# Attention scores on two row tiles of the TensorE array: q without zero rows, the two heads' products next to each other

## The chip, the cores and the metric

One Trainium2 chip; the kernel runs on 1 of its cores as one launch. The metric is the device time of that launch in microseconds (us). Engines by their names in the profile: PE is TensorE (matrix products), PEld its weight loads, DVE is VectorE, ACT is ScalarE, POOL is GpSimd, and SP is the engine that issues nearly all DMAs here.

## The reference

Three stages follow each other. The change touches the first.

```python
# q, k, v: batch 4, 8 heads, 768 rows, head size 64, f32; n_sink 4, window 128
scores = scale * np.matmul(q, k.transpose(0, 1, 3, 2))
keep = is_sink | in_window             # the first 4 keys, and the last 128
scores = np.where(keep, scores, -1e9)
a = np.exp(scores - max);  a = a / (sum + 1e-9)
x = a @ v                              # -> 3072 tokens x 512
# dense layer: h = x @ w_in; y = (h * cos(h)) @ w_out      (512 -> 2048 -> 512)
# routing to one of 8 experts, then relu(y @ w1[e]) @ w2[e], times its gate
```

## The kernel before

The 32 heads are worked in 16 pairs. Both heads of a pair lie on top of each other: the 128 partitions of `k_sb` hold k transposed of head 0 in partitions 0 to 63 and of head 1 in 64 to 127. `qz` holds q transposed twice as wide, `[128, 2, 768]`: in the part for head 0 the partitions 64 to 127 are zero, in that for head 1 the partitions 0 to 63. So each head's scores are a product over all 128 partitions, half of whose terms are zero. The zeros are written once by two DVE memsets (L793), and the loads (L395) put the values beside them, one DMA for each head.

A pair has six steps, i = 0 to 5, one for each block of 128 query rows. A step computes scores against the block's own keys and the block before (128 columns for i = 0, 256 else), and for i from 2 on against 32 sink columns too ("wide" steps, 288 columns). The order on PE is written out by hand in `attention` (L1247): the scores of step n (L1185, sinks L1187), then, where there are sinks to add, the turn of the packed sink probabilities of step n-3 (L1205), the turn of the probabilities of step n-2 (L1197), the product with v of step n-3 (L1219), and the sink product (L1230). The last two sorts fall in steps i = 0 and i = 2. A matrix product in f32 shows as two MATMULs in the trace, each with a weight load of its own (192 score products of 128 or 256 columns, 384 MATMULs); a turn shows as one.

L1219 works on half of the array's columns: head 0 fills the 64 output partitions 0 to 63, head 1 those from 64 on (128*64 in the trace). All other products of this stage use the whole array (128*128).

DVE in step n: the denominators and reciprocals of step n-1 (L861, L863) as soon as ACT's two exponentials of that step are done, scaling of its first head (L865), masking with row maximum of step n (L839, one for each head), in steps i = 0 and 2 the copy of the turned sinks (L854), the copy of the turned probabilities of step n-2 (L847), and in steps i = 2 and 5 half of a weight split for the next stage (L872). ACT in step n: scaling of the second head of step n-1 (L623), two exponentials (L606), in i = 1 and 4 a weight split (L593), in odd steps the copy of a finished block (L618).

Scores go to three PSUM banks in turn, so the scores of head h of step n wait until the mask of three products earlier has read its bank (`masked_made`). SP loads a pair's k, q, v and four sink pieces of v (L391 to L403) once the sinks of that buffer's last pair are weighed (step i = 2 of the pair after it), and PE takes them up three steps later, at i = 0 (`qkv_loaded`).

Of the kernel before, what the change touches and what calls it, by code (L numbers as in the profile page):

```python
# [24 lines left out]
P = 128  # L25
# [6 lines left out]
def at_least(engine, semaphore, value):  # L32

    if isinstance(value, int) and value <= 0:
        return
    engine.wait_ge(semaphore, value)


def build_program(nc, qT, kT, v, config, w_dense, modality, w_gate, modality_bias, w_expert, out):
    PAIRS, _, S = qT.shape  # L40
    HD = 64
# [4 lines left out]
    SINK = 32  # L46
# [16 lines left out]
    STEPS = 2 * QB  # L63
# [9 lines left out]
    with ctx:  # L73
        def sb(name, shape, dt=F32, where=ctx):
            return where.enter_context(nc.sbuf_tensor(name, shape, dt))

        def sem(name):
            return ctx.enter_context(nc.semaphore(name))
# [21 lines left out]


        with ExitStack() as a:
            qz = [sb(f"qz{i}", [P, 2, S], where=a) for i in range(2)]
            k_sb = [sb(f"k_sb{i}", [P, S], where=a) for i in range(2)]
            v_sb = [sb(f"v_sb{i}", [P, QB, P], where=a) for i in range(2)]
            v_sink = [sb(f"v_sink{i}", [P, 2 * P], where=a) for i in range(2)]
            x_stage = [sb(f"x_stage{i}", [P, S], where=a) for i in range(2)]
            masked = [sb(f"masked{i}", [P, 2, WIDE], where=a) for i in range(2)]
            probs = [sb(f"probs{i}", [P, 2, WIDE], where=a) for i in range(4)]
            probsT = [sb(f"probsT{i}", [P, 2, 2 * P], where=a) for i in range(2)]  # L110
            sink_probs = [sb(f"sink_probs{i}", [P, 4, SINK], where=a) for i in range(2)]
            sink_probsT = sb("sink_probsT", [P, P], where=a)
            neg_max = sb("neg_max", [P, 2 * STEPS], where=a)
            sums = sb("sums", [P, 2 * STEPS], where=a)
            den = sb("den", [P, 2 * STEPS], where=a)
            rden = sb("rden", [P, 2 * STEPS], where=a)

            rel, below, keep = (x_stage[0][:, 2 * P * i:2 * P * (i + 1)] for i in range(3))
            col, is_sink = (x_stage[1][:, P * i:P * (i + 1)] for i in range(2))
            mask0 = sb("mask0", [P, P], where=a)  # L120
            mask1 = sb("mask1", [P, 2 * P], where=a)
            mask2 = sb("mask2", [P, 2 * P + SINK], where=a)
# [100 lines left out]
        ident_cleared = sem("ident_cleared")  # L223
        consts_made = sem("consts_made")
        mask_step = sem("mask_step")
        q_zeros_made = sem("q_zeros_made")
        sink_zeros_made = sem("sink_zeros_made")
        qkv_loaded = [sem(f"qkv_loaded{i}") for i in range(2)]
        raw_loaded = [sem(f"raw_loaded{i}") for i in range(2)]
# [2 lines left out]
        scores_done = sem("scores_done")  # L232
        masked_made = sem("masked_made")
# [115 lines left out]
        def columns_of(i):  # L349

            return (P, 2 * P) if i == 0 else (0, 2 * P if i == 1 else WIDE)
# [6 lines left out]
        S_BANK, T_BANK, O_BANK, X_BANK = bank[0:3], bank[3:5], bank[5:7], bank[7]  # L358
# [13 lines left out]
        def _(sp):  # L372
# [14 lines left out]
            def load_pair(it, i):  # L387

                at_least(sp, sinks_weighed, 2 * SG * (it - 1) + SG * (i + 1))
                pair = 2 * it + i  # L390
                sp.dma_start(k_sb[i][:, :], kT[bass.ds(pair, 1), :, :].rearrange("o p s -> (o p) s")).then_inc(qkv_loaded[i], 16)  # L391
                if isinstance(it, int) and it == 0:
                    sp.wait_ge(q_zeros_made, i + 1)
                for h in range(2):
                    sp.dma_start(qz[i][HD * h:HD * (h + 1), h, :],  # L395
                                 qT[bass.ds(pair, 1), HD * h:HD * (h + 1), :].rearrange("o p s -> (o p) s"),
                                 ).then_inc(qkv_loaded[i], 16)
                sp.dma_start(v_sb[i][:, :, :].rearrange("p n d -> p (n d)"),
                             v[bass.ds(pair, 1), :, :].rearrange("o p s -> (o p) s")).then_inc(qkv_loaded[i], 16)
                if isinstance(it, int) and it == 0:  # L400
                    sp.wait_ge(sink_zeros_made, i + 1)
                for u in range(4):
                    sp.dma_start(v_sink[i][SINK * u:SINK * (u + 1), HD * u:HD * (u + 1)],  # L403
                                 v[bass.ds(pair, 1), 0:SINK, HD * (u % 2):HD * (u % 2 + 1)].rearrange("o p s -> (o p) s"),
                                 ).then_inc(qkv_loaded[i], 16)
                load_piece(it, i)
# [73 lines left out]
        def _(pool):  # L480
# [34 lines left out]
                    pack_all(it)  # L515
            with pool.Else():
                for i in range(2):
                    pool.wait_ge(qkv_loaded[i], 128)
                pool.memset(any_q[:, :, :], 0.0).then_inc(any_zeros, 1)
                pool.iota(any_rel[:, :], pattern=[[-1, S]], base=0, channel_multiplier=1,  # L520
                          allow_small_or_imprecise_dtypes=True).then_inc(any_zeros, 1)
                pool.iota(any_sink[:, :], pattern=[[1, S]], base=0, channel_multiplier=0,
                          allow_small_or_imprecise_dtypes=True).then_inc(any_zeros, 1)
# [259 lines left out]
        def _(dve):  # L783
# [5 lines left out]
                ins.then_inc(mask_step, 1)  # L789
                dve.wait_ge(mask_step, done[0])  # L790

            for i in range(2):
                dve.memset(qz[i][:, :, :], 0.0).then_inc(q_zeros_made, 1)  # L793
            dve.wait_ge(config_loaded, 16)
            halves = cfg_lo[:, :].rearrange("p (a b) -> p a b", b=2)
            dve.tensor_copy(halves[:, :, 0:1], cfg_i[:, :].bitcast(U32).rearrange("p (a b) -> p a b", b=2)[:, :, 0:1]).then_inc(mask_step, 1)
# [218 lines left out]
            n = link(dve.tensor_scalar(chain2[:, :], chain2[:, :], 1.0, None, ALU.min))  # L1015
            after(n)
            for m, x in enumerate((bsel, bpart)):
                n = link(dve.tensor_tensor(x, bias_sb[:, m:m + 1, :].broadcast_to(full), wide(is_mod[:, m, :], full), ALU.mult))
# [25 lines left out]
            n = link(dve.tensor_tensor(weighed[:, :, :], logits[:, :, :], wide(top[:, :], full), ALU.is_equal))  # L1044
# [9 lines left out]
            def by_tile(x):  # L1054
# [14 lines left out]
            n = link(dve.tensor_reduce(in_use[:, 0::2, :].rearrange("p a e -> p e a"),  # L1069
                                       over[:, :, :].rearrange("p e (i a) -> p e a i", a=2), AX.X, ALU.add))  # L1070
# [102 lines left out]
        def _(pe):  # L1173

            def scores(it, n):
                par, i = n // QB, n % QB
                if i == 0:
                    pe.wait_ge(qkv_loaded[par], 128 * it + 128)
                for h in range(2):

                    at_least(pe, masked_made, 2 * STEPS * it + 2 * n + h - 2)
                    to = S_BANK[(2 * n + h) % 3]
                    q = qz[par][:, h, i * P:(i + 1) * P]
                    lo, hi = columns_of(i)
                    last = pe.matmul(to[:, lo:2 * P], q, k_sb[par][:, (i - 1) * P + lo:(i + 1) * P], start=True, stop=True)  # L1185
                    if hi > 2 * P:
                        last = pe.matmul(to[:, 2 * P:hi], q, k_sb[par][:, 0:SINK], start=True, stop=True)  # L1187
                    last.then_inc(scores_done, 1)

            def turn_probs(it, m):  # L1190
                pe.wait_ge(scaled_first, STEPS * it + m + 1)
# [324 lines left out]
```

## Time and profile before

| | |
|---|---|
| median of 3 runs | 1204.07 us (1203.34 to 1204.21) |
| profiled execution, span | 1203.8 us |
| attention | 8.85 us (first scores) to about 256 us |
| dense layer | from 260.2 us |
| PE busy over the span | 1145.4 us (95%) |
| granted TensorE clock, mean | 0.978 |

The span, from the first to the last instruction, is all that the profile has of its execution's time; the median of the timed runs stands 0.3 us above it. All times in the rows below are microseconds from the start of the span. "Idle before <-releaser" is how long the engine had nothing to do before such an instruction, and what ended that.

### The profile page before, as it was taken

What the parts mean: (1) busy time and instruction counts of PE and PEld (TensorE: products, weight loads), DVE (VectorE), ACT (ScalarE), POOL (GpSimd) and SP (SyncE); (2) the same over time, 40 slices, a digit from 0 to 9 for tenths busy, and PEclk for the clock granted to TensorE, in tenths of its full rate; (3) what the DMA queues carried; (4) which work ended last, traced back from release to release, by engine and by line L of the source; (5) the groups of instructions that cost most, each with busy time, mean ns of one, the idle gap of its engine ahead of it and who ended that gap; (6) DMA issues with size and microseconds to landing.
All of it is one profiled execution on the core that took longest, in us unless ns stands there. A gap on an engine that the chain in (4) does not pass through costs nothing.

```text
span 1203.8 us, 20823 instructions
## 1 busy us (share of the span) xinstructions
PE 1145.4 (95%) x6588; PEld 961.5 (80%) x6589; DVE 618.9 (51%) x1522; ACT 493.6 (41%) x1099; POOL 86.7 (7%) x174
## 2 busy tenths in 40 slices
PE   6999999989999999999999999997599999999996
PEld 5777777768888888888888888886589999899895
DVE  7888888854454444444345445445773222252221
ACT  5777777753333333333334334332352221241221
POOL 0000000000000000000000000000111121221121
PEclk9999999989999999999999999998599999999998
DMA  5444444510001002002002000000573111121110
GB/s 118 143 142 142 142 142 142 173 67 1 1 9 63 1 0 70 0 0 70 0 0 70 0 0 36 1 1 35 193 257 111 35 52 36 36 105 52 35 50 18
DMA packets 33993, 76.61 MB, mean 64 GB/s; under 512 B 10398, under 2 KB 10398, under 8 KB 33952
## 3 DMA queue, kind: packets, MB, share of 16 engines
q1 hardware_dynamic: 29312, 63.50, 17.1%
q0 software_dynamic: 4640, 12.59, 3.1%
q8 instruction: 22, 0.36, 0.1%
q14 instruction: 19, 0.16, 0.0%
HBM read 58.77 MB, written 19.92 MB: 65 GB/s over the span
## 4 chain that ended last, share of the span: by engine, by line
PE 86%; DVE 4%; issue 3%; DMA 3%; SPq 2%; ACT 1%; POOL 0%; DVEq 0%; POOLq 0%; ACTq 0%
PE bank L1310 23%; PE bank L1324 22%; PE bank L1450 14%; PE bank L1438 12%; PE bank L1185 4%; DMA v_sink<-v_n 3%; PE bank L1219 2%; PE bank L1230 2%; PE bank L1197 2%; PE bank L1342 1%; PE bank L1420 1%; SPq L403 1%; PE bank L1411 1%; SPq L395 1%; PE bank L1187 1%
## 5 line engine op out<-in xcount | busy, mean ns | idle before, releaser
L1310 PE MATMUL bank<-x_hi,w_hi 128*128 128x512 f32 x384 | 156.1, 406 | 4.7 <-issue 4.2
L1310 PE MATMUL bank<-x_lo,w_hi 128*128 128x512 f32 x384 | 153.0, 399 | 0.0
L1310 PE MATMUL bank<-x_hi,w_lo 128*128 128x512 f32 x384 | 152.7, 398 | 0.0
L1324 PE MATMUL bank<-w_hi,g_hi 128*128 128x512 f32 x384 | 152.3, 397 | 0.4 <-DVE g_lo L986 0.4
L1324 PE MATMUL bank<-w_hi,g_lo 128*128 128x512 f32 x384 | 152.1, 396 | 0.0
L1324 PE MATMUL bank<-w_lo,g_hi 128*128 128x512 f32 x384 | 151.8, 395 | 0.0
L1145 DVE SCALAR_TENSOR_TENSOR h_lo<-bank,h_hi 128x256 fp32r<-128x256 f32 x112 | 47.6, 425 | 173.4 <-ACT h_hi L756 172.2
L1450 PE MATMUL bank<-xg_hi,w_hi 128*128 128x256 f32 x448 | 127.7, 285 | 4.3 <-DVE xg_lo L1139 2.8
L974 DVE TENSOR_SCALAR whole<-turns 128x512 f32<-128x512 f32 x96 | 41.0, 427 | 175.4 <-ACT turns L707 175.4
L1185 PE MATMUL bank<-k_sb,qz 128*128 128x256 f32 (+1 forms) x384 | 114.7, 400 | 16.8 <-DMA v_sink<-v_n 16.8
L707 ACT ACTIVATE turns<-bank 128x512 f32<-128x512 f32 x96 | 57.5, 599 | 177.7 <-PE bank L1310 177.7
L1450 PE MATMUL bank<-xg_hi,w_lo 128*128 128x256 f32 x448 | 128.1, 286 | 0.0
L1450 PE MATMUL bank<-xg_lo,w_hi 128*128 128x256 f32 x448 | 127.6, 285 | 0.0
L756 ACT ACTIVATE h_hi<-bank 128x256 fp32r<-128x256 f32 x112 | 43.2, 386 | 187.1 <-PE bank L1450 182.0
L606 ACT ACTIVATE probs<-masked,neg_max 128x288 f32<-128x288 f32 (+1 forms) x192 | 96.5, 503 | 35.1 <-DVE neg_max L839 25.3
L712 ACT ACTIVATE cosine<-frac 128x512 f32<-128x512 f32 x96 | 60.7, 632 | 114.2 <-DVE frac L977 114.2
L986 DVE TENSOR_TENSOR g_lo<-g_sb,g_hi 128x512 fp32r<-128x512 f32 x96 | 66.5, 693 | 65.0 <-ACT g_hi L717 64.5
L982 DVE TENSOR_TENSOR g_sb<-bank,cosine 128x512 f32<-128x512 f32 x96 | 66.4, 692 | 64.0 <-ACT cosine L712 63.5
L1450 PEld LDWEIGHTS bank<-xg_hi,w_hi 128*128 128x128 f32 x448 | 85.7, 191 | 9.4 <-issue 5.6
L1310 PEld LDWEIGHTS bank<-x_hi,w_hi 128*128 128x128 f32 x384 | 72.9, 190 | 21.3 <-issue 4.4
L717 ACT ACTIVATE g_hi<-g_sb 128x512 fp32r<-128x512 f32 x96 | 60.7, 632 | 71.1 <-DVE g_sb L982 71.1
L1450 PEld LDWEIGHTS bank<-xg_lo,w_hi 128*128 128x128 f32 x448 | 86.0, 192 | 3.5
(159 smaller groups left out, 2087.8 us busy)
## 6 DMA issues: line engine op xcount, KB each, us to landing
raw<-w_expert SPq DMA_DIRECT2D x32, 512.0 KB, 4.9
raw<-w_dense SPq DMA_DIRECT2D x16, 512.0 KB, 4.5
k_sb<-k_t SPq DMA_DIRECT2D x16, 384.0 KB, 3.3
qz<-q_t SPq DMA_DIRECT2D x32, 192.0 KB, 4.0
v_sb<-v_n SPq DMA_DIRECT2D x16, 384.0 KB, 4.4
xT_scratch<-x_stage SPq DMA_DIRECT2D x16, 384.0 KB, 4.6
x_raw<-xT_scratch SPq DMA_DIRECT2D x6, 1024.0 KB, 5.1
y_scratch<-y_sb SPq DMA_DIRECT2D x6, 1024.0 KB, 4.3
```

The source lines that it names most:

```text
L606: act.activation(probs[n % 4][:, h, lo:hi], masked[n % 2][:, h, lo:hi], ACT.Exp, scale=-1.0, bias=neg_max[:, 2 * n + h:2 * n + h + 1], acc ...
L707: act.activation(turns[:, :], H_BANK[f % 2][:, :], ACT.Copy, scale=INV_2PI, bias=0.25).then_inc(turns_made, 1)
L712: act.activation(cosine[:, :], frac[:, :], ACT.Sin, scale=TWO_PI).then_inc(cos_made, 1)
L717: act.activation(g_hi[f % 4][:, :], g_sb[:, :], ACT.Copy).then_inc(g_hi_made, 1)
L982: dve.tensor_tensor(g_sb[:, :], H_BANK[f % 2][:, :], cosine[:, :], ALU.mult).then_inc(g_made, 1)
L986: dve.tensor_tensor(g_lo[f % 4][:, :], g_sb[:, :], g_hi[f % 4][:, :].bitcast(F32), ALU.subtract).then_inc(g_lo_made, 1)
L1145: dve.scalar_tensor_tensor(out=h_lo[f % 4][:, :], in0=EH_BANK[f % 2][:, 0:TT], scalar=0.0, in1=h_hi[f % 4][:, :].bitcast(F32), op0=ALU.max ...
L1185: last = pe.matmul(to[:, lo:2 * P], q, k_sb[par][:, (i - 1) * P + lo:(i + 1) * P], start=True, stop=True)
L1310: last = pe.matmul(H_BANK[f % 2][:, :], a[:, w], b[:, k, :], start=x == 0, stop=x == 3 * KD - 1)
L1324: last = pe.matmul(Y_BANK[t][:, :], a[f % 4][:, t * P:(t + 1) * P], b[:, w], start=f == 0 and x == 0, stop=f == FB1 - 1 and x == 2)
L1438: last = pe.matmul(EY_BANK[j][:, :], a[f % 4][:, j * P:(j + 1) * P], b[:, w], start=f == 0 and x == 0, stop=f == FB2 - 1 and x == 2)
L1450: last = pe.matmul(EH_BANK[f % 2][:, 0:TT], a[:, w], b[:, k, :], start=x == 0, stop=x == 3 * KD - 1)
```

## The change

`qz` becomes `q_sb`, `[128, 768]`: each head's q in its own 64 partitions, loaded by one DMA. The two memsets go, and with them the wait of SP for them. Each head's product now contracts over its own 64 partitions, the weights and the moving operand both taken from those: head 0 on rows 0 to 63 of the array, head 1 on rows 64 to 127. Both heads' window products are issued, then both heads' sink products. The wait for a free bank stands once, ahead of both heads: for the mask of head 0 of the step before.

```diff
-            qz = [sb(f"qz{i}", [P, 2, S], where=a) for i in range(2)]
+            q_sb = [sb(f"q_sb{i}", [P, S], where=a) for i in range(2)]
...
-                if isinstance(it, int) and it == 0:
-                    sp.wait_ge(q_zeros_made, i + 1)
-                for h in range(2):
-                    sp.dma_start(qz[i][HD * h:HD * (h + 1), h, :],
-                                 qT[bass.ds(pair, 1), HD * h:HD * (h + 1), :].rearrange("o p s -> (o p) s"),
-                                 ).then_inc(qkv_loaded[i], 16)
+                sp.dma_start(q_sb[i][:, :], qT[bass.ds(pair, 1), :, :].rearrange("o p s -> (o p) s")).then_inc(qkv_loaded[i], 16)
...
-            for i in range(2):
-                dve.memset(qz[i][:, :, :], 0.0).then_inc(q_zeros_made, 1)
...
-                    pe.wait_ge(qkv_loaded[par], 128 * it + 128)
+                    pe.wait_ge(qkv_loaded[par], 112 * it + 112)
+                at_least(pe, masked_made, 2 * STEPS * it + 2 * n - 1)
+                lo, hi = columns_of(i)
+                to = [S_BANK[(2 * n + h) % 3] for h in range(2)]
+                rows = [slice(HD * h, HD * (h + 1)) for h in range(2)]
+                last = [None, None]
                 for h in range(2):
-
-                    at_least(pe, masked_made, 2 * STEPS * it + 2 * n + h - 2)
-                    to = S_BANK[(2 * n + h) % 3]
-                    q = qz[par][:, h, i * P:(i + 1) * P]
-                    lo, hi = columns_of(i)
-                    last = pe.matmul(to[:, lo:2 * P], q, k_sb[par][:, (i - 1) * P + lo:(i + 1) * P], start=True, stop=True)
-                    if hi > 2 * P:
-                        last = pe.matmul(to[:, 2 * P:hi], q, k_sb[par][:, 0:SINK], start=True, stop=True)
-                    last.then_inc(scores_done, 1)
+                    last[h] = pe.matmul(to[h][:, lo:2 * P], q_sb[par][rows[h], i * P:(i + 1) * P],
+                                        k_sb[par][rows[h], (i - 1) * P + lo:(i + 1) * P], start=True, stop=True)
+                if hi > 2 * P:
+                    for h in range(2):
+                        last[h] = pe.matmul(to[h][:, 2 * P:hi], q_sb[par][rows[h], i * P:(i + 1) * P],
+                                            k_sb[par][rows[h], 0:SINK], start=True, stop=True)
+                for h in range(2):
+                    last[h].then_inc(scores_done, 1)
```

PE, a step i = 2 with its sinks, before: head 0 (window, sinks), then head 1, and behind them the rest of the step. The size is that of the output, partitions by columns; a row is one product.

```order
L1185 MATMUL bank<-k_sb,qz 128x256 [waits masked_made]
L1187 MATMUL bank<-k_sb,qz 128x32
L1185 MATMUL bank<-k_sb,qz 128x256 [waits masked_made]
L1187 MATMUL bank<-k_sb,qz 128x32
L1205 MATMUL bank<-ident,sink_probs 128x128 [waits sinksT_made,sinks_packed]
L1197 MATMUL bank<-ident,probs 128x128 [waits probsT_made,scaled_second,scaled_first]
L1197 MATMUL bank<-ident,probs 128x128
L1219 MATMUL bank<-probsT,v_sb 64x128 [waits probsT_made]
L1219 MATMUL bank<-probsT,v_sb 64x128 x3
L1230 MATMUL bank<-sink_probsT,v_sink 128x128 [waits sinksT_made]
```

The same step now (L1177 and L1181 are the scores; L1193, L1201, L1215, L1226 the rest):

```order
L1177 MATMUL bank<-k_sb,q_sb 128x256 [waits masked_made]
L1177 MATMUL bank<-k_sb,q_sb 128x256
L1181 MATMUL bank<-k_sb,q_sb 128x32 x2
L1201 MATMUL bank<-ident,sink_probs 128x128 [waits sinksT_made,sinks_packed]
L1193 MATMUL bank<-ident,probs 128x128 [waits probsT_made,scaled_second,scaled_first]
L1193 MATMUL bank<-ident,probs 128x128
L1215 MATMUL bank<-probsT,v_sb 64x128 [waits probsT_made]
L1215 MATMUL bank<-probsT,v_sb 64x128 x3
L1226 MATMUL bank<-sink_probsT,v_sink 128x128 [waits sinksT_made]
```

The second head's window product has moved ahead of the first head's sink product, one of the two waits is gone, and nothing behind the scores has moved.

SP, the load of a pair in the loop, before:

```order
L391 ISA [waits sinks_weighed]
L391 DMA k_sb<-k_t 128x768
L395 DMA qz<-q_t 64x768
L395 ISA
L395 DMA qz<-q_t 64x768
L398 DMA v_sb<-v_n 128x768
L403 DMA v_sink<-v_n 32x64
```

And now:

```order
L390 ISA [waits sinks_weighed]
L390 DMA k_sb<-k_t 128x768
L391 DMA q_sb<-q_t 128x768
L392 DMA v_sb<-v_n 128x768
L397 DMA v_sink<-v_n 32x64
```

One DMA with both heads stands in the place of two, and everything behind it is one issue earlier.

## Rows read from the trace of the kernel before

**Rows 1.** The page: busy time, and one line of the 40 slices.
```profile
PE 1145.4 (95%) x6588; PEld 961.5 (80%) x6589; DVE 618.9 (51%) x1522; ACT 493.6 (41%) x1099; POOL 86.7 (7%) x174
...
DVE  7888888854454444444345445445773222252221
```

**Rows 2.** Stretches: PE, PEld, DVE, ACT, POOL busy; clock; DMA share; GB/s.
```profile
40.00:240.00 200.00, 191.00 (x1520) 154.14 (x1519) 178.07 (x682) 147.95 (x458) 12.39 (x52) 1.00 0.48 143
258.00:268.00 10.00, 7.79 (x22) 6.18 (x23) 1.12 (x2) 2.21 (x3) 2.02 (x12) 0.66 0.38 122
```

**Rows 3.** Waits from 40 to 240 us, DVE: us in total, times, longest.
```profile
DVE masked L839 <- PE bank L1185: 4.9, 16, 0.5
DVE masked L839 <- PE bank L1187: 2.5, 13, 0.2
```

**Rows 4.** Waits from 40 to 240 us, PE.
```profile
PE bank L1185 <- DMA v_sink<-v_n: 7.5, 12, 1.3
PE bank L1230 <- DVE sink_probsT L854: 1.4, 4, 0.5
```

**Rows 5.** Chain, steps i = 1 and i = 2 on PE: start, us, what.
```profile
101.94 0.87 PE bank L1185 x4
102.81 0.44 PE bank L1197 x4
103.24 0.59 PE bank L1219 x8
103.83 0.63 PE bank L1185 x2
104.46 0.14 PE bank L1187 x2
104.60 0.51 PE bank L1185 x2
105.11 0.14 PE bank L1187 x2
105.25 0.14 PE bank L1205
...
106.20 0.72 PE bank L1230 x4
```

**Rows 6.** Timeline of PE: a product with v of two blocks only.
```profile
245.55 0.44 PE L1219 MATMUL bank<-probsT,v_sb 128*64 128x128 f32 x4
245.92 0.70 PE L1185 MATMUL bank<-k_sb,qz 128*128 128x256 f32 x2
```

**Rows 7.** Chain, from one wide step's denominators to the next's.
```profile
18.04 0.18 DVE den L861
...
19.22 1.16 ACT probs L606 x4
20.40 0.18 DVE den L861
```

**Rows 8.** Chain at the start of the kernel.
```profile
1.12 1.35 DVE qz L793
...
2.48 0.57 SPq L395
...
3.72 0.59 SPq L398
...
5.75 3.05 DMA v_sink<-v_n
```

**Rows 9.** Timeline of SP at the start: start, us, what.
```profile
1.18 0.42 SPq L391 DMA_DIRECT2D k_sb<-k_t  x1
```

**Rows 10.** Timeline of SP, a pair's load in the loop.
```profile
107.10 0.33 SPq L391 DMA_DIRECT2D k_sb<-k_t  x1
107.53 1.19 SPq L395 DMA_DIRECT2D qz<-q_t  x2
```

**Rows 11.** Chain, the end of that load.
```profile
110.98 3.54 DMA v_sink<-v_n
```

More of the change, by code:

```diff
@@ L225, in build_program @@
         mask_step = sem("mask_step")
-        q_zeros_made = sem("q_zeros_made")
         sink_zeros_made = sem("sink_zeros_made")
@@ L517, in _ @@
                 for i in range(2):
-                    pool.wait_ge(qkv_loaded[i], 128)
+                    pool.wait_ge(qkv_loaded[i], 112)
                 pool.memset(any_q[:, :, :], 0.0).then_inc(any_zeros, 1)
```

## The prediction, made before the changed kernel ran

> **What bounds the kernel now.** I read the busy line and the slices first [rows 1]: PE is busy 95% of the span, but in the first eight slices, the attention, DVE stands at 7 to 8 tenths and falls to 4 behind them. So a shorter PE there is not simply a shorter kernel. The stretch from 40 to 240 us says it in numbers [rows 2]: PE busy 191.0 of 200 us, DVE 178.1, ACT 148.0, at full granted clock. PE is the longest, DVE has 11% left.
>
> Next the waits. DVE waited for scores 4.9 us in 16 waits for L1185 and 2.5 us in 13 for L1187, together 7.4 us in 200 [rows 3]. That is what late scores cost DVE. PE itself waited 7.5 us for a pair's load and 1.4 us for DVE's copy of the sinks [rows 4]. Both engines wait for each other a little: the stage is balanced, not plainly PE-bound. The wide steps show the third bound, a loop through two engines: denominators of one step, reciprocal, scaling, mask, two exponentials (1.16 us), denominators of the next, from 18.04 to 20.40 = 2.36 us [rows 7], with PE nowhere in it. A pair of six steps takes about 15.2 us now ((256 - 8.85) / 16 less the last steps' tail); six such loops would be 14.2 us, and DVE's weight split and sink copies lengthen some of them. So even with PE for nothing a pair could lose 1 us at most, 16 us in all.
>
> **What the scores cost on PE, part by part.** In step i = 1 the four score MATMULs of 256 columns take 0.87 us, 0.217 each; the four turns of 128 columns 0.44, 0.11 each [rows 5]. In a wide step the first head takes 0.63 + 0.14, the second 0.51 + 0.14, together 1.42 us [rows 5]. Two MATMULs of 256 columns would be 0.43. The first head's 0.63 holds 0.20 more: it follows L1219, which uses half of the columns, and the array has to be empty before its division changes, with the weight load bare behind it. The second head's 0.51 holds 0.08: its weight load had only the 32-column product to hide under. A sink product's 0.14 is the bare load of its second weights.
>
> Do two tiles of the array work at the same time? The trace has them in columns. L1219 has 8 MATMULs of 128 columns, and takes 0.59 us, not 8 x 0.11 = 0.88 [rows 5]; with 4 it takes from 245.55 to 245.92, 0.37 [rows 6]. The difference is 0.22 for four more MATMULs, so two slots of 0.11: both heads run side by side, and what is left over, 0.59 - 0.43 = 0.37 - 0.22 = 0.15, is the change of division. If rows do as columns do, a wide step's scores take what one head takes: 0.63 + 0.14 = 0.77, and 0.65 us is saved; in i = 1 0.43, in i = 0 0.22 (by 128 columns). Per pair 4 x 0.65 + 0.43 + 0.22 = 3.25 us.
>
> The Trainium skill speaks to this in "TensorE: Matmul & The Clock Gate", "Part 3: Packing small matmuls": matmuls start and end in strict program order. By that rule head 1's first pass could only start with head 0's second, and two passes of two heads would take three slots, not two; L1219 with 4 MATMULs would then take 0.15 + 3 x 0.11 = 0.48. The trace has 0.37 [rows 6] and disagrees, for column tiles. I keep the rule as a rival for row tiles.
>
> **What is added on PE.** Before, scores and turns used the same division, and the turn's weights loaded under the scores. Now the array changes its division behind the scores in all six steps, and ahead of the scores also in the two steps that follow a sink product (i = 1 and 3); in the others L1219 stands ahead, whose change is paid already. No row shows a change from or to a division by rows. The nearest are 0.20 (columns to whole) and 0.15 (whole to columns) [rows 5]. Bounds: nothing, and twice 0.20. I take 0.20, less the 0.08 that the turn's load costs bare behind a sink product already: 4 x 0.12 + 2 x 0.20 behind, 2 x 0.20 ahead, 1.28 us per pair. PE's net: 3.25 - 1.28 = 1.97 us less per pair, some 13.2 of 15.2.
>
> In "TensorEngine Tiling (Array Packing)", "Key Properties", the Trainium skill states that changing the tiling mode drains the engine. The 0.20 behind L1219 agrees [rows 5]; a price for rows it does not give.
>
> **What of it reaches the end.** Only what DVE and ACT waited for. The 7.4 us of waits stand in 200 us, the attention has 242: 9.0 us. Those for L1187 (2.5) are the wide steps' second head, whose scores now come 0.65 us earlier: all of it goes. Those for L1185 (4.9) are steps i = 0 and 1, where head 0's scores are the late ones. Head 0 needs its own two passes as before, 0.43 us at i = 1, and now 0.20 more ahead of them. What helps there is only that PE comes to them earlier, from its slack. Both ends: none of it, all of it. I take a quarter, 1.2, since the entry stands against it and the load of the pair keeps PE late at i = 0. Then 3.7 us of 200, 4.5 us of 242. Ends for this term: 2.5 x 1.21 = 3.0 and 9.0.
>
> The bank wait. Head 0's scores now wait for the mask of head 0 of the step before, not for one mask earlier. That mask ends long before: behind it PE has turns, L1219 and mostly more, at least 1.03 us [rows 5]. Cost nothing; behind it would stand everything on PE. Had PE no such work, it would be 0.5 us a step.
>
> **The loads.** SP issues one q DMA for two. In the loop two take 1.19 us [rows 10], so about 0.6 us goes; k's, of 128 partitions, takes 0.33. The last sink piece lands 3.54 us after SP is done [rows 11], and the whole chain, 107.10 to 114.52, is 7.4 us against three steps i = 3 to 5. It becomes 6.8, while those three steps get shorter by some 0.3. PE waits for it now [rows 4], with DVE mostly at work meanwhile. Taken at nothing, 0 to 1.5 us gain. The bytes are the same.
>
> At the start it counts. k's issue ends at 1.60 [rows 9]; the first q issue waits for the memset until 2.48 [rows 8]. It can now start at 1.64, 0.84 earlier, and one issue of 0.57 + 0.04 is gone: 1.45 us. The rest of the chain, v, the sink pieces and 3.05 us of landing [rows 8], moves with it. Late next would be DVE's masks; they start earlier too, by up to the second memset, and had over 1 us to spare. From there the attention runs in its loop, so I count all of it: 1.45 us, at worst 0.8.
>
> **Sum.** 1203.8 (span) - 4.5 - 1.45 = 1197.85; the median of the timed runs stands 0.3 above the span: 1198.1 us. By the ends of the terms: 1203.8 - 3.0 - 0.8 + 0.3 = 1200.3, and 1203.8 - 9.0 - 1.45 - 1.5 + 0.3 = 1192.2.
>
> **Rivals.**
>
> *Three slots, not two.* Head 1's first pass beside head 0's second only. For: same program order, and row tiles are not column tiles. Against: [rows 6]. PE saves 4 x 0.33 + 0.21 + 0.11 = 1.64 and pays 1.28, nearly nothing; but both heads' scores then come after 0.20 + 0.64 + 0.33 where head 0's came after 0.77, so the mask of head 0 waits up to 0.4 us. In the balanced loop I put 0.3 us a pair on that: 1203.8 + 4.8 - 1.45 + 0.3 = 1207.5.
>
> *The tiles take turns* (slower). The row tiles share what feeds the array, the passes stand one behind the other, and only the changes of division are left, 1.28 us per pair on the engine that is longest: +20.5 us, 1203.8 + 20.5 - 1.45 + 0.3 = 1223. The point from which PE is longer than now: less than 1.28 / 3.25 = 40% of the possible overlap.
>
> *DVE and ACT set the pace.* PE gets short and the loop of 2.36 us and DVE's 178 of 200 us [rows 2, 7] take over at once; of the waits half comes back as waits on ACT. Then some 1.8 us instead of 4.5: 1200.8.
>
> *Clock.* From 258 to 268 us the granted clock is 0.66 [rows 2], a stretch at 1.2 GHz after PE's pause before the dense layer. With more pauses inside the attention such a stretch could come there, or this one be longer or shorter: 3 us either way. Before, pauses of up to 1.3 us [rows 4] left the clock at 1.00.
>
> **Chances.** Forecast (1192 to 1200.3) 0.45; DVE and ACT at once (1200 to 1202.5) 0.15; three slots (1202.5 to 1209) 0.18; turns (over 1209) 0.16; clock, half to each side, 0.06. The range 1191 to 1209 leaves out 0.19. The forecast's own range is 1192 to 1200.3. Faster by over 0.2% (2.4 us, about what a measurement here tells from no change) is below 1201.7: 0.45 + 0.12 + 0.03 = 0.60. Within 0.2%, to 1206.5: 0.03 + 0.10 = 0.13. Slower: 0.27.
>
> **What would show it.** Right: the two heads' L1177 MATMULs start nearly together, a wide step's scores take about 0.77 us; the turns behind start some 0.2 us late; PE busy in the attention near 13.2 us a pair with idle time in front of turns and products that wait for DVE and ACT; DVE's waits for the sink products gone, those at i = 0 and 1 left; first scores at 7.4 us. Wrong: starts of the second head 0.2 us or more behind the first (three slots or turns), bubbles at the division well over 0.2, DVE idle more than before, or the same step time with PE waiting (the loop).

## The result: the changed kernel is slower, 1210.56 us

| | before | changed |
|---|---|---|
| median of 6 runs | 1204.14 us (1202.98 to 1206.34) | 1210.56 us (1207.36 to 1215.46) |
| ratio to before | | 1.005, 95% interval 1.003 to 1.007 |
| profiled execution, span | 1203.8 us | 1208.9 us |
| mean granted clock | 0.978 | 0.973 |

The page, PE against [rows 1]: 24 us less busy, 5 us more span.

```profile
PE 1121.7 (93%) x6588; PEld 925.9 (77%) x6589; DVE 612.8 (51%) x1520; ACT 491.4 (41%) x1099; POOL 86.5 (7%) x174
```

**The products run as forecast.** The timeline of PE, a wide step i = 2 with its sinks (start, us, line; L1177 and L1181 scores, L1201 and L1193 turns, L1215 product with v):

```profile
246.15 0.70 PE L1177 MATMUL bank<-k_sb,q_sb 64*128 64x256 f32 x4
246.69 0.31 PE L1181 MATMUL bank<-k_sb,q_sb 64*128 64x32 f32 x4
246.93 0.33 PE L1201 MATMUL bank<-ident,sink_probs 128*128 128x128 f32 x1
247.09 0.38 PE L1193 MATMUL bank<-ident,probs 128*128 128x128 f32 x2
247.40 0.66 PE L1215 MATMUL bank<-probsT,v_sb 128*64 128x128 f32 x8
```

From the first score to the sinks' turn it is 0.78 us. The timeline of the kernel before has 1.33 for the same stretch, both heads one behind the other:

```profile
103.76 0.70 PE L1185 MATMUL bank<-k_sb,qz 128*128 128x256 f32 x2
104.30 0.30 PE L1187 MATMUL bank<-k_sb,qz 128*128 128x32 f32 x2
104.44 0.68 PE L1185 MATMUL bank<-k_sb,qz 128*128 128x256 f32 x2
104.95 0.30 PE L1187 MATMUL bank<-k_sb,qz 128*128 128x32 f32 x2
105.09 0.31 PE L1205 MATMUL bank<-ident,sink_probs 128*128 128x128 f32 x1
```

The two heads' first MATMULs start 0.007 us apart: both heads work side by side. From the scores to the product with v it is 1.25 us, where it was 105.55 - 103.76 = 1.79; the 0.54 gained are close to the forecast's 0.65 - 0.12 = 0.53. The change of division behind the scores costs 0.09 us: the turn starts 0.20 us after the last score MATMUL starts, where it was 0.11.

**What PE saved it waits.** The waits from 40 to 240 us, PE then DVE (us in total, times, longest):

```profile
PE bank L1226 <- DVE sink_probsT L846: 23.5, 25, 1.4
...
PE bank L1177 <- DMA v_sink<-v_n: 4.0, 6, 1.2
```

```profile
DVE masked L831 <- PE bank L1177: 7.9, 13, 1.5
...
DVE masked L831 <- PE bank L1181: 2.8, 2, 1.7
```

PE's wait for DVE's copy of the sinks was 1.4 us in 4 waits [rows 4], now 23.5 in 25. DVE's waits for scores, 4.9 and 2.5 before [rows 3], are not less. But these 200 us hold two stretches at a lower clock (below), and the two waits for L1181 lie in one of them. From 60 to 209 us both kernels ran at full clock. DVE there, now and then before:

```profile
DVE den L853 <- ACT probs L600: 7.8, 28, 0.4
DVE masked L831 <- PE bank L1177: 4.1, 9, 0.5
```

```profile
DVE den L861 <- ACT probs L606: 4.0, 19, 0.2
DVE masked L839 <- PE bank L1185: 2.8, 10, 0.4
DVE masked L839 <- PE bank L1187: 1.9, 10, 0.2
```

The waits for the sink scores are gone, as forecast; those for the window scores grew from 2.8 to 4.1 us, and DVE waits 3.8 us more for ACT. Each waits for the other. A step i = 2 to 3 on DVE, and PE's part between, from the timeline:

```profile
106.61 0.46 DVE L831 CUSTOM_DVE_ANT_0 masked<-bank,mask 128x288 f32<-128x288 f32 x1
...
107.38 0.29 DVE L846 COPY sink_probsT<-bank 128x128 f32<-128x128 f32 x1
...
109.42 0.46 DVE L831 CUSTOM_DVE_ANT_0 masked<-bank,mask 128x288 f32<-128x288 f32 x1
```

```profile
107.72 0.71 PE L1226 MATMUL bank<-sink_probsT,v_sink 128*128 128x128 f32 x4 [0.79 <-DVE sink_probsT L846]
108.36 0.70 PE L1177 MATMUL bank<-k_sb,q_sb 64*128 64x256 f32 x4
...
109.13 0.66 PE L1193 MATMUL bank<-ident,probs 128*128 128x128 f32 x4
```

It is a loop: two masks (from 106.61, the second read out at 107.38), the sink copy behind them, the sink product (from 107.72), the next step's scores queued behind that (108.36, done about 109.3), the next mask at 109.42: 2.81 us, of which PE's own work is 1.4 and no other work of PE is in it. In steps i = 0 and 2 PE can be as fast as it likes in everything else. DVE's scaling of the first head, at the end of its own chain with ACT, ends only a little earlier here, at 109.28, so this timeline alone doesn't settle which chain binds; e5 below does. From the masks' starts, two pairs in the middle (101.56 to 132.08) take 30.52 us, 15.26 each; before, 100.22 to 130.63 is 15.21 each (15.27 and 15.24 over the pairs 4 to 15 that hold no fall of the clock). The steady attention gained nothing.

**What made it slower is the clock.** Stretches of the changed kernel (columns as in [rows 2]; the eighth number is the granted clock):

```profile
40.00:240.00 200.00, 167.29 (x1489) 122.54 (x1491) 170.63 (x665) 143.93 (x449) 11.86 (x50) 0.97 0.41 135
```

```profile
21.50:55.60 34.10, 28.22 (x264) 20.59 (x264) 30.12 (x119) 24.98 (x79) 2.13 (x9) 1.00 0.39 127
55.70:59.00 3.30, 3.30 (x14) 2.09 (x16) 1.74 (x9) 1.00 (x4) 0.00 (x0) 0.50 0.02 5
59.20:209.20 150.00, 123.58 (x1148) 90.70 (x1144) 131.35 (x512) 111.11 (x346) 9.49 (x40) 1.00 0.43 142
209.30:219.40 10.10, 10.00 (x51) 7.17 (x51) 5.94 (x23) 4.83 (x16) 0.24 (x1) 0.50 0.00 0
```

Twice inside the attention TensorE stood at 1.2 GHz, for 3.4 and 10.2 us; before it stood at 2.4 GHz from 40 to 240 us [rows 2]. Ahead of the first fall PE had waited 1.27 us for the sink copy. Ahead of the second it had been busy 1.78 of 3.2 us, waiting for the pair's load and then for the sink copy:

```profile
55.56 1.17 PE L1226 MATMUL bank<-sink_probsT,v_sink 128*128 128x128 f32 x4 [1.27 <-DVE sink_probsT L846]
```

```profile
206.00:209.20 3.20, 1.78 (x17) 1.25 (x17) 3.08 (x14) 2.32 (x9) 0.47 (x2) 1.00 0.58 225
```

A third slow stretch stands at the start, and it is no fall: both kernels begin at the lower rate, and the changed one keeps it longer. The granted clock of the profile reads 1.00 there in both, so this is read from the durations. Four turns take 0.66 us at full clock; the timeline of the changed kernel has them at nearly twice that until about 21.5 us:

```profile
18.07 1.11 PE L1193 MATMUL bank<-ident,probs 128*128 128x128 f32 x4
...
21.59 0.66 PE L1193 MATMUL bank<-ident,probs 128*128 128x128 f32 x4
```

Before, the same four took 0.63 at 15.18 us already, and the products came to full rate at about 13.4 us. Between its first scores and 12 us the changed kernel's PE had paused 0.55 and 0.76 us for masks; in the kernel before it was busy without a break from 8.85 to 15 us. In the profiled runs of this case the four kernels with zero rows come to full rate between 13.4 and 15.0 us, the ten with row tiles between 17.3 and 22.9. That the pauses are the reason is not shown.

From mask to mask, the three pairs that hold these stretches took 15.59, 16.40 and 19.00 us, the same pairs before 13.88, 15.30 and 15.28: 1.7 + 1.1 + 3.7 = 6.5 us lost, the 1.7 of them in the first pair by the late rise. Against that stands the start, where the first scores came at 7.93 us and not 8.85. The net, 5.6, is the 5.1 us of the spans within half a microsecond. The runs agree: at a mean clock of 0.976 and 0.975 they took 1207.5 and 1207.4 us, at 0.973 to 0.970 1210.3 to 1211.7, at 0.967 1215.5.

### The profile page after: what moved, and what is told of

Its sections match the earlier page's. It is cut to its first block, busy times and chain, and to the rows that moved or that the text cites. A ratio compares the mean times of both kernels' runs of the same rounds, so it can differ in the third digit from the quotient of the medians.

```text
span 1208.9 us, 20700 instructions
## 1 busy us (share of the span) xinstructions
PE 1121.7 (93%) x6588; PEld 925.9 (77%) x6589; DVE 612.8 (51%) x1520; ACT 491.4 (41%) x1099; POOL 86.5 (7%) x174
## 4 chain that ended last, share of the span: by engine, by line
PE 79%; DVE 8%; issue 6%; ACT 4%; DVEq 1%; POOL 1%; DMA 0%; ACTq 0%; SPq 0%; POOLq 0%
PE bank L1306 22%; PE bank L1320 22%; PE bank L1446 14%; PE bank L1434 12%; ACT probs L600 3%; PE bank L1177 2%; PE bank L1338 1%; PE bank L1226 1%; PE bank L1416 1%; DVE rden L855 1%; DVE den L853 1%; DVE w_lo L864 1%; DVE probsT L839 1%; DVE masked L831 1%; PE bank L1407 1%
## 5 line engine op out<-in xcount | busy, mean ns | idle before, releaser
L1177 PE MATMUL bank<-k_sb,q_sb 64*128 64x256 f32 (+1 forms) x384 | 69.1, 439 | 21.1 <-DMA v_sink<-v_n 13.1
```

What stands on the lines that cost most here:

```text
L1177: last[h] = pe.matmul(to[h][:, lo:2 * P], q_sb[par][rows[h], i * P:(i + 1) * P], k_sb[par][rows[h], (i - 1) * P + lo:(i + 1) * P], start=T ...
```

## The experiments

Each was timed beside the kernel before on the same chip, but not all on one chip, so the ratios compare better than the medians. "A pair" is the mean of the pairs 4 to 15 from the masks' starts of the profiled run, for the changed kernel, e4 and e12 without those that hold a fall of the clock. The last two rows include them.

| | a pair, us | clock, 40 to 240 us | median, us | ratio to before (95%) |
|---|---|---|---|---|
| before | 15.24 | 1.00 | 1204.1 to 1204.8 | 1 |
| changed | 15.27 | 0.97 | 1210.56 | 1.005 (1.003 to 1.007) |
| e1 fill, columns | 15.26 | 1.00 | 1205.95 | 1.001 (1.0001 to 1.0019) |
| e2 fill, whole | 15.26 | 1.00 | 1205.64 | 1.0006 (0.9998 to 1.0015) |
| e10 fill elsewhere | 15.28 | 1.00 | 1204.57 | 1.000 (0.9992 to 1.0009) |
| e3 order alone | 15.64 | 1.00 | 1210.54 | 1.0045 (1.0032 to 1.0058) |
| e4 tiles, old order | 15.26 | 0.95 | 1209.7 | 1.004 (1.0026 to 1.0055) |
| e12 turn first alone | 15.27 | 0.99 | 1210.85 | 1.0071 (1.0043 to 1.0098) |
| e9 before, sinks first | 14.91 | 1.00 | 1197.94 | 0.9943 (0.9931 to 0.9956) |
| e5 sinks first | 14.69 | 1.00 | 1196.31 | 0.9928 (0.9915 to 0.9942) |
| e6 sinks late | 14.62 | 1.00 | 1195.39 | 0.9923 (0.9909 to 0.9936) |
| e11 late, early load | 14.62 | 1.00 | 1195.11 | 0.992 (0.9907 to 0.9933) |
| e7 sinks late, filled | 16.41 | 0.91 | 1220.37 | 1.0121 (1.0102 to 1.0139) |
| e8 before, sinks late | 17.18 | 0.97 | 1229.67 | 1.0206 (1.0191 to 1.0221) |

### Is it the clock? Fill PE's pauses

e1: two more products ahead of the wait for the sinks, on half of the array's columns.

```diff
             def weigh_sinks(it, m):
                 par, _ = group_of(m)
+                for c in (2 * P, P):
+                    pe.matmul(O_BANK[m // 2 % 2][0:HD, 2 * P:2 * P + c], ident[:, 0:HD], v_sb[par][:, 4:4 + c // P, :].rearrange("p n d -> p (n d)"), start=False, stop=False)
                 pe.wait_ge(sinksT_made, sink_group(it, m) + 1)
```

> The changed kernel with two extra products on PE ahead of each wait for DVE's copied sinks (L1226), 256 and 128 columns onto half of the array's columns, some 0.64 us of work where PE waited 0.94 us on average. They add values of v to PSUM columns that nothing reads; the result is unchanged. Theory 1 (the clock): a steady pair of the changed kernel takes as long as before (15.2 to 15.3 us both), and what makes it slower are stretches at 1.2 GHz inside the attention that come because PE idles; with the idle filled the granted clock stays at 1.00 from 10 to 250 us, and the time is 1203 (1201 to 1205). Theory 2 (PE's added switches in the loop through DVE): the filling changes nothing, 1208 to 1212, and the falls of the clock, where there are any, are as many.

1205.95 us, 4.6 less than the changed kernel with 1.28 us more work a pair on PE. The clock held from 40 to 240 us in the profiled run, and in all 11 runs the mean clock was that of the kernel before or more (0.978 to 0.981; before 0.978 to 0.980, changed kernel 0.967 to 0.976). A mean of 0.978 alone does not rule out one short fall: the profiled run of e12 has it too, with two falls of 3.4 us before 244 us. The stretch, and PE's wait:

```profile
40.00:240.00 200.00, 181.84 (x1630) 133.63 (x1628) 174.68 (x682) 147.15 (x459) 12.34 (x52) 1.00 0.44 144
```

```profile
PE bank L1228 <- DVE sink_probsT L846: 7.0, 12, 0.8
```

The pair stays at 15.26 us. Theory 1 holds; 1206 is 1 us over the expected range.

e2 is e1 with the whole array, `O_BANK[m // 2 % 2][:, 2 * P:2 * P + c]` from `ident[:, :]`.

> The same filling, but on the whole array: besides the activity it moves the array's change from column tiles to the whole array from behind the wait for DVE to ahead of it, about 0.1 us less between the copied sinks and the next scores, 32 times. Theory 1: clock 1.00, 1 to 3 us below e1_fill_columns, near 1200 to 1203. Theory 2: as theory 1 says of the 32 times 0.1, but from 1210: 1205 to 1209, with the clock as in the changed kernel.

1205.64 us: the clock as e1, but the 1 to 3 us of an earlier change of division are not there (0.3, within the spread). That part was wrong: 15.26 us a pair again.

e10 puts as much filling behind the product with v in the other steps:

```diff
                 last.then_inc(window_weighed, 1)
+                if i % 2 == 0:
+                    pe.matmul(O_BANK[m // 2 % 2][0:HD, 2 * P:4 * P], ident[:, 0:HD],
+                              v_sb[par][:, 4:6, :].rearrange("p n d -> p (n d)"), start=False, stop=False)
```

> The changed kernel with as much filling as e1 (1.28 us a pair, half of the array's columns, onto PSUM columns that nothing reads), but behind the product with v in steps i = 1, 3 and 5, not in front of the wait for the copied sinks in i = 0 and 2. If PE's mean activity makes the clock fall, it is held as in e1, 1204 to 1207; if the pauses at the pair's start do (0.6 us for the load and 1.0 us for the copied sinks within some 3 us), the falls stay as in the changed kernel, mean clock 0.967 to 0.976 and 1207 to 1215.

1204.57 us, mean clock 0.978 to 0.980 in 11 runs. The waits for the sink copy stayed, and the clock held all the same:

```profile
PE bank L1229 <- DVE sink_probsT L846: 19.4, 27, 1.2
```

So it is not the pauses by themselves. PE's total does not tell the kernels apart clearly either: in e11 below PE is busy 169 of 200 us, hardly more than in e12 (168, with a fall) and in the changed kernel (167; at full clock, from 60 to 209 us, 125.9 in e11 and 122.8), in pauses of at most 0.8 us, and its clock is 1.00. Ahead of both falls of the changed kernel little work and a pause of over 1 us stood together (PE busy 1.91 us from 52.3 to 55.7, 1.78 from 206.0 to 209.2). Which of the two a fall needs, these runs don't tell.

### Order and tiles apart

e3: the kernel before, with only the order and the one wait of the change (`q = qz[par][:, h, ...]`, over 128 partitions).

```diff
+                at_least(pe, masked_made, 2 * STEPS * it + 2 * n - 1)
...
                 for h in range(2):
-                    at_least(pe, masked_made, 2 * STEPS * it + 2 * n + h - 2)
...
+                    last[h] = pe.matmul(to[h][:, lo:2 * P], qz[par][:, h, i * P:(i + 1) * P],
+                                        k_sb[par][:, (i - 1) * P + lo:(i + 1) * P], start=True, stop=True)
+                if hi > 2 * P:
+                    for h in range(2):
+                        last[h] = pe.matmul(to[h][:, 2 * P:hi], qz[par][:, h, i * P:(i + 1) * P],
+                                            k_sb[par][:, 0:SINK], start=True, stop=True)
...
```

> The kernel before, q with zero rows, two q DMAs and the memsets, with only the order and the single bank wait of the change: window products of both heads, then sinks of both, over the whole array. PE's work is as before, so both theories expect the clock as before. If the order or the wait costs something by itself, head 0's scores come 0.14 to 0.65 us later in wide steps (both heads done at once instead of one after the other) and it shows here: up to 0.4 us a pair more in steps where DVE has no slack, 1204 to 1212. If they cost nothing, 1204.

1210.54 us, 15.64 a pair with a full clock. The scores of a step i = 2, and DVE's waits from 40 to 240 us:

```profile
121.29 1.13 PE L1184 MATMUL bank<-k_sb,qz 128*128 128x256 f32 x4
122.26 0.53 PE L1188 MATMUL bank<-k_sb,qz 128*128 128x32 f32 x4
122.62 0.31 PE L1208 MATMUL bank<-ident,sink_probs 128*128 128x128 f32 x1
```

```profile
DVE masked L839 <- PE bank L1188: 6.4, 19, 0.4
DVE masked L839 <- PE bank L1184: 4.3, 15, 0.4
```

Head 0's last sink MATMUL ends 1.27 us after the step's first score starts (122.56 - 121.29), where it was 0.84 (104.60 - 103.76), and the mask waits: 10.7 us in 200 against 7.4. The order alone costs 0.4 us a pair; two tiles side by side give it back. I had priced the order at nothing.

e4: row tiles with the order and waits of before.

```diff
-                at_least(pe, masked_made, 2 * STEPS * it + 2 * n - 1)
...
                 for h in range(2):
...
+                    at_least(pe, masked_made, 2 * STEPS * it + 2 * n + h - 2)
+                    rows = slice(HD * h, HD * (h + 1))
+                    q = q_sb[par][rows, i * P:(i + 1) * P]
```

> The changed kernel (row tiles, one q DMA, no memsets) with the order and the two waits of before: head 0 window and sinks, head 1 window and sinks. If tiles run side by side whatever stands between them in program order, a wide step's scores still take about 0.77 us and the time is that of the changed kernel, 1207 to 1212; if matmuls start in program order, head 1's window starts behind head 0's sinks, about 0.43 + 0.1 us later, a step's scores take 1.2 us or more, PE idles less, and by theory 1 the clock falls less often; by theory 2 it is slower than the changed kernel, over 1212.

1209.7 us, with a clock of 0.95 between 40 and 240 us. A wide step's scores:

```profile
61.33 0.71 PE L1178 MATMUL bank<-k_sb,q_sb 64*128 64x256 f32 x4
61.87 0.31 PE L1180 MATMUL bank<-k_sb,q_sb 64*128 64x32 f32 x4
62.11 0.66 PE L1190 MATMUL bank<-ident,probs 128*128 128x128 f32 x4
```

0.78 us again, although head 0's sink product stands ahead of head 1's window product in program order: the first window MATMULs of the two heads start 0.014 us apart, at 61.333 and 61.347. In one wide step of a pair, i = 5, head 1 starts 0.3 to 0.4 us behind, but there its own wait, for the mask of head 0 of the step before, holds it. So these tiles of different rows do not wait for each other's order; this was the first of its two expectations, and it settles the rival of three slots.

### Open the loop

e5: the sinks turned ahead of the step's scores, and DVE's copy ahead of its scaling and masks.

```diff
 # PE, attention
                 for n in range(STEPS):
+                    at = lagged(it, n, PV_LAG)
+                    if at and at[1] % 2 == 1 and group_of(at[1])[1] > 0:
+                        turn_sinks(*at)
                     scores(it, n)
...
 # PE, attention_step
-                if sinks:
-                    turn_sinks(*at)
...
 # DVE, attention: the copy_sinks(*at) that stood behind mask_scores(it, n) now stands ahead of scale_first
```

> The changed kernel, with the sinks turned on PE ahead of the step's scores, and copied by DVE ahead of its scaling and masks (steps i = 0 and 2): the sink product no longer waits behind both masks. Theory A (in the steady state the loop mask, sink copy on DVE, sink product, next scores on PE sets steps i = 0 to 3, and that is where the gain went): a pair takes 14.7 to 14.95 us and not 15.25; without falls of the clock that is 5 to 9 us less than e1's 1206, 1197 to 1201, with falls as in the changed kernel 1201 to 1207. Theory B (DVE and ACT's own loop sets the steps whatever PE does): 15.2 to 15.3 a pair still, 1207 to 1212.

1196.31 us, 14.69 a pair, mean clocks 0.979 and 0.980 in 5 runs. The timeline of the sink product, with no wait in front, and of the masks of i = 2 and 3:

```profile
116.17 0.71 PE L1226 MATMUL bank<-sink_probsT,v_sink 128*128 128x128 f32 x4
...
116.31 0.46 DVE L831 CUSTOM_DVE_ANT_0 masked<-bank,mask 128x288 f32<-128x288 f32 x1
...
118.77 0.46 DVE L831 CUSTOM_DVE_ANT_0 masked<-bank,mask 128x288 f32<-128x288 f32 x1
```

2.46 us where it was 2.81, and the sink product starts before the masks begin. Over nine pairs, against e10, which has the changed kernel's steps and a held clock, the median from mask to mask is 2.04 us and not 2.51 from step i = 0 to 1, 2.46 and not 2.81 from i = 2 to 3, and 2.91 and not 2.71 from i = 5 to the next i = 0, where the copy now stands ahead of the masks. The two steps that the loop should hold are the two that got shorter. Theory A holds, theory B falls; the time is 0.7 us under the range for a held clock.

e12 is e5 without the move on DVE.

> Half of e5: the changed kernel with the sinks turned ahead of the scores on PE, DVE's copy still behind the masks. Theory A says that the place of the copy behind both masks is what closes the loop: the sink product still waits, 15.2 to 15.4 us a pair, falls of the clock as in the changed kernel, 1207 to 1213. If the turn was what came late, it is as fast as e5, 1196.

1210.85 us (1205.79 to 1222.44 in 12 runs, mean clocks 0.959 to 0.978), 15.27 a pair. As theory A said: the copy's place behind the masks closes the loop, not the turn's. PE busy is 168 of 200 us:

```profile
40.00:240.00 200.00, 168.44 (x1508) 121.39 (x1508) 173.89 (x679) 146.58 (x457) 12.34 (x52) 0.99 0.43 141
```

e9: the edit of e5 on the kernel before.

> The kernel before (zero rows, whole array, one head behind the other) with the sinks turned ahead of the scores and copied by DVE ahead of scaling and masks, the edit of e5, which leaves the pair's load where it was. If PE's own work bound the kernel before (15.2 us a pair), 15.0 to 15.3 a pair and 1200 to 1206; the rest to e5's 1196.3 is what the row tiles are worth once the loop is open, some 0.3 to 0.5 us a pair and 1 us at the start. If it comes down to 1197 too, the row tiles are worth only the start, and the loop through the copied sinks was the bound of both kernels.

1197.94 us, 14.91 a pair. It missed the expected 1200 to 1206 and came near its other branch, 1197: the loop through the copied sinks bound the kernel before too. DVE's waits for scores from 40 to 240 us are all but gone, with PE's products as they were:

```profile
DVE masked L839 <- PE bank L1187: 1.1, 6, 0.2
DVE masked L839 <- PE bank L1185: 0.7, 3, 0.3
```

PE is the full engine now, busy 194 of 200 us where e5's is busy 177:

```profile
40.00:240.00 200.00, 194.48 (x1559) 157.44 (x1557) 182.66 (x701) 151.80 (x469) 12.62 (x53) 1.00 0.49 144
```

So with the loop open the row tiles do gain in the steady attention: e5 takes 0.22 us a pair less than e9, some 3 us over the pairs. The medians are only 1.6 us apart. In the profiled runs e5 loses 1.2 us of it in the first pair (15.29 us against 14.12), where its products come to full rate at about 20.5 us and e9's at 14.3.

e6: the sink product one step later, behind the next step's scores.

```diff
             def attention_step(it, n):
                 at = lagged(it, n, PV_LAG)
+                late = lagged(it, n, PV_LAG + 1)
+                if late and late[1] % 2 == 1 and group_of(late[1])[1] > 0:
+                    weigh_sinks(*late)
...
-                if sinks:
-                    weigh_sinks(*at)
...
```

> The changed kernel, with the sink product issued one step later, behind the next step's scores: the loop through DVE's sink copy is opened, and PE changes its division twice less a pair (0.2 us each). The pair's load then starts about 1 us later. Theory A: 14.7 to 14.95 us a pair where the load is not late; PE idles more than in the changed kernel, so the clock falls at least as often: 1199 to 1208 with a spread of some us. Theory B: 15.2 to 15.3 a pair, 1207 or more. If the load becomes the bound, waits of PE for DMA stand at every i = 0 and the pair is 15.0 to 15.4.

1195.39 us, 14.62 a pair, the clock 1.00 from 40 to 240 us. PE waited 10.4 us for loads in 200, and DVE for no scores at all, so that cost nothing (e11 below removes these waits and is no faster).

e7 is e6 with e1's filling behind the product with v; e8 is the kernel before with the sink product late.

> e6 with the filling of e1 (0.64 us of PE work, twice a pair, behind the product with v of i = 3 and 5, onto PSUM columns that nothing reads). Theory 1 (PE's idling makes the clock fall): granted clock 1.00 in the attention and a mean of 0.978 or more, and the time e6 would have without falls: by theory A 1196 to 1201. If the falls come from something else they stay, and it is as e6 or slower.

> The kernel before (zero rows, whole array, its order) with the sink product one step later, as e6. If the loop through the sink copy bound the kernel before too, it gets faster, to 15.0 a pair and 1200 to 1203; if PE bound it (15.2 us of work a pair, of which this takes nothing but the waits for the sinks), 1203 to 1206. The difference to e6 and e7 is what the row tiles are worth once the loop is open: by theory A with the clock held 3 to 6 us, by theory B nothing.

1220.37 and 1229.67 us (ratios 1.0121 and 1.0206): both missed, and for one reason, that a later sink product starts the pair's load later. PE's waits from 40 to 240 us, of e7 and of e8:

```profile
PE bank L1177 <- DMA v_sink<-v_n: 22.4, 12, 3.2
```

```profile
PE bank L1185 <- DMA v_sink<-v_n: 22.2, 11, 2.3
```

There the load became the bound; at the pairs' starts PE stood still up to 3.2 us, and the clock fell (0.91 and 0.97 in the same stretch). e7 says nothing on filling, then, and e8 nothing on what tiles are worth; e10 and e9 answer these.

e11: e6 with the loads of k and q tied to the pair's last scores.

```diff
-                at_least(sp, sinks_weighed, 2 * SG * (it - 1) + SG * (i + 1))
+                at_least(sp, scores_done, 2 * STEPS * (it - 1) + 2 * QB * (i + 1))
                 sp.dma_start(k_sb[i][:, :], ...)
                 sp.dma_start(q_sb[i][:, :], ...)
+                at_least(sp, sinks_weighed, 2 * SG * (it - 1) + SG * (i + 1))
                 sp.dma_start(v_sb[i][:, :, :], ...)
```

> e6 with the loads of k and q started when the pair's last scores are done, not when its sinks are weighed; v and the sink pieces wait as before. e6's PE waited 10.4 us for the load in 200 us, up to 1.1 each. If those waits reach DVE, 1193 to 1195; if DVE and ACT set the 14.6 us a pair, the waits go and the time stays at 1195.4 within 0.7.

1195.11 us (1193.27 to 1195.47), the fastest version, 0.8% under before; against e6 no difference that can be told. The waits for the load are gone, what is left is waiting for masks:

```profile
40.00:240.00 200.00, 169.34 (x1592) 125.60 (x1590) 181.46 (x713) 155.03 (x481) 13.12 (x55) 1.00 0.44 142
```

```profile
PE bank L1178 <- DVE neg_max L832: 30.6, 68, 0.8
```

## Why the prediction was wrong

*The cost of the scores and two slots: right; the change of division: priced too high.* A wide step's block takes 0.78 us against the 0.77 forecast. A change of division costs 0.09 us from one MATMUL's start to the next (0.20 against 0.11), behind the scores and ahead of them alike, not 0.12 and 0.20: the 0.20 of [rows 5] holds the load that stands bare without a change too. PE was busy 122.8 us from 60 to 209 us, before 142.6: some 2.0 us less a pair, the forecast's 1.97, though from 14.6 and not from 15.2, since a pair held some waiting of PE already. And e4 shows the tiles side by side whatever the order. The rivals of three slots and of tiles that take turns are out.

*"What of it reaches the end": the step that failed.* I took DVE's 7.4 us of waits for scores as PE's lateness, and let the wide steps' part of it go and a quarter of the rest, 4.5 us. But scores come late to DVE mostly because the sink product in front of them waits for DVE's own copy, behind DVE's own masks. That loop was in the profile: [rows 4] has the wait for `sinksT` with 1.4 us in 4 waits, which looked small only because PE arrived there hardly earlier than the copy. The part for L1187 did go, but the waits for L1177 and for ACT grew in its place (4.1 and 7.8 us from 60 to 209 us, before 2.8 and 4.0). In place of 4.5 us the steady attention gained nothing, 15.27 a pair against 15.24. e9 shows what the loop cost before: without it, 6.9 us less with PE's products untouched.

*The order at nothing: wrong in part.* I judged the one wait, not the order. Head 0's scores come 0.4 us later when the array is one (e3, 6.1 us); with tiles side by side they come when they came before.

*The start, 1.45 us: mis-sized.* SP came to its last piece 1.8 us earlier, but that landed after 3.90 us and not 3.05 [rows 8], and the first scores came 0.92 us earlier:

```profile
3.99 3.90 DMA v_sink<-v_n
...
7.93 0.85 PE bank L1177 x4
```

Nor did all of it last, as I had counted: by the masks of the second pair the changed kernel was 0.8 us behind (24.51 against 23.72). In that first pair its products came to full rate 8 us later.

*The clock: the rival with 0.06 that decided the sign.* I had named the mechanism, more pauses inside the attention, and set against it that pauses of 1.3 us had left the clock alone. What the kernel before had was single pauses in dense work. The changed one pauses for the copied sinks in nearly every step i = 0 and 2 (25 times in 13 pairs), ahead of the second fall 1.7 us after a pause for the load. The two falls cost 4.8 us of the profiled run and the late rise at the start 1.7, where I had put 3 us on either side; e1 and e10, which only add work to PE, take 4.6 and 6.0 us off. Filling did not bring the rise back to where it was: in e1 and e10 it came at 17.3 and 18.6 us, and their first pairs took 14.05 and 15.16 us, before 13.88.

*DVE and ACT at once: half right.* The 2.36 us loop holds steps i = 3 to 5; with the sink loop open they and DVE's other work set 14.6 us a pair (in e11 DVE waits for no scores), where I had put the floor at 14.2.

So the sign came from the clock, and the missing gain from the loop. Both were shown by runs. Open are two things: why the kernels with row tiles come to full rate later at the start, and where between e10 and the changed kernel the clock begins to fall.

## What to carry to other kernels

When two engines wait a little for each other, follow one such wait round: if it comes back to the engine that waits, making the other one faster gives nothing, and moving the one copy that closes the loop may give everything (here 6.9 us for two moved calls). Before making TensorE's work shorter where it isn't the bound, ask what it will do with the time: here the shorter work gained nothing, and two falls of the clock took 4.8 us. Packing two heads in row tiles is sound and cost 0.09 us at each change of the array's division; it gained only where TensorE's own work was last (0.22 us a pair, e5 against e9).

## What the runs showed of the hardware

- Row tiles of 64 partitions run side by side in f32 with full overlap: 4 MATMULs of 256 columns take 0.54 us from the first's start to the sinks' (246.15 to 246.69), as 2 did before (103.76 to 104.30), also where other products of one tile stand between in program order (e4).
- Each change between whole array, column tiles and row tiles adds 0.09 us, from one MATMUL's start to the next.
- Adding useless work made a kernel faster: 1.28 us more of products a pair on half of the array's columns, 4.6 to 6.0 us less in all (e1, e10).
- The granted clock of 200 us was 1.00 with PE busy 169.3 us in even pauses (e11), and 0.99 and 0.97 at 168.4 and 167.3 us in uneven ones (e12, the changed kernel; their slow stretches count in).
- TensorE begins at half rate in every kernel here, though the profile's granted clock reads 1.00; full rate comes at 13.4 to 15.0 us with zero rows and at 17.3 to 22.9 us with row tiles.
- A DMA chain that is issued sooner isn't done sooner by as much: SP came to the last issue 1.8 us earlier, the data landed 0.9 us earlier.
